# Transposes and logits moved into the last attention round; the attention's tiles laid anew over the experts' weights

## The chip, the cores and the metric

One core of one Trainium2 chip. The metric is the device time of one execution in microseconds, the median of the runs shown. The kernel before took 555.84 us (555.8 to 557.96 in three runs).

## The reference

Three layers follow one another: a linear attention with a decaying state (4 batches, 8 heads, 768 tokens, head size 48), a mixture of experts in which every slot is a weighted mean of all tokens (3072 tokens, 384 wide, 8 experts of 4 slots, 1024 hidden), and a squared-ReLU layer (2048 hidden).

```python
for t in range(S):                                   # attention, y: [B, H, S, D]
    cur = einsum('bhd,bhe->bhde', u[None] * kt, vt)
    y[:, :, t] = einsum('bhd,bhde->bhe', rt, state + cur)
    state = wt[:, :, :, None] * state + einsum('bhd,bhe->bhde', kt, vt)
x = y.transpose(0, 2, 1, 3).reshape(B * S, H * D)    # [3072, 384]
logits = x @ phi                                     # [3072, 32]
d = softmax of logits over the tokens                # max over axis 0
slot_input = (d.T @ x).reshape(E, S_per_e, D)
slot_out[e] = relu(slot_input[e] @ w1[e]) @ w2[e]
x = (softmax of logits over the slots) @ slot_out
h = relu(x @ w_in); out = (h * h) @ w_out
```

## The kernel before

The attention runs in eight rounds (`ROUNDS`), each of four heads of one batch in two sets `s` of two heads. A round turns its inputs (r, k, w) on TensorE into two banks `tbank` (`turn_inputs`, L402), which ScalarE copies out (`inputs_out`, L743); it then works in six levels per set (`level`, L451 for the levels 1 to 3, L468 for 0, 4 and 5), between which VectorE scales the tiles (`update`, L1041) and merges products (`merge`, L1063) and ScalarE widens operands (`widen`, L802). The order on every engine is written out by hand. While round `rd` works through its levels, the inputs of round `rd + 1` are turned and the rest of round `rd - 1` is finished: k turned (`turn_k`, L415; out by `k_out`, L773), k times v (`k_times_v`, L432; out by `kv_out`, L781), the scan over chunks (`scan`, VectorE, L1070), the near and the far product (`y_near`, L485; `y_far`, L501), and the copy to the tile `X` (`y_to_x`, L818). The nine `next_inputs` places of the last round are empty, since no round follows.

Behind the last level the rest of the last round stands alone. Between its steps TensorE turns x (`turn_x`, L559: 24 uses of three 128x128 transposes each, in 4 banks, evacuated by ScalarE, L891, and VectorE, L1102, in turns). Twenty uses concern columns of earlier rounds, and four need the last round. Then come the logits (L583: 24 products of 384 columns, each executed as two matmul instructions, four 32-column groups of the array side by side), their copy (L904), the maximum over tokens (L1105, turned by L594), both softmaxes, the slots (L605), the experts' first product with `w1_sb` (L623, all eight experts), and their second product in two halves: `down(0)` with `w2_lo`, `down(1)` with `w2_hi` (both L646; `down(1)` waits for a quarter of `w2_hi` before each quarter of its steps). The squared-ReLU layer (L707 to L709) takes the rest of the span.

Weights come by DMA, 1.5 MB for one expert's w1. ScalarE's queue issues `w1` (`load_w1`, L237): experts 0 to 2 in the rounds 0 to 2; experts 3 to 5 in the last round behind the first levels, and 6 and 7 at its end. SP's queue issues `w2_lo[3]` when the last y is in `X` (L335), `w2_lo[0:3]` after the logits (L337), `w_in` (L339), and `w2_hi` in 16 pieces (L343). `w1_sb` lies over the attention's tiles, so an expert can be loaded only when the tiles under it are done with. Before, behind the three early experts lie nat, rt, rk2, rk0 and wl, in this order (the end of wl0 is past expert 7); `x_t`, where the turned x goes, begins behind the eighth expert and so lies over the rest of wl0, wl1, aa0, wide, k_tok and the first of rk1, of which the last round uses several.

## Time and profile before

| | |
|---|---|
| median of three runs | 555.84 us |
| the profiled execution | 555.19 us, span 553.4 us, mean granted clock 0.953 |
| TensorE busy | 485.5 us (88%) |
| VectorE / ScalarE busy | 334.6 us (60%) / 332.8 us (60%) |
| shares of the chain that ended last | PE 72%, ACT 11%, issue 7%, SPq 4%, DVE 4% |
| attention | to about 264 us; mixture of experts to about 320 us; squared-ReLU layer to the end |

In the profile a busy share tells how long an engine had work, not what the end waited for; for that there is the chain of waits, which is followed back from the last instruction. "issue" in it is time in which an engine waited for nothing that the profile shows. The granted clock is a share of TensorE's full speed: 1.00 is 2.4 GHz and 0.50 is 1.2 GHz.

### The profile page before, as it was taken

How to read it: one execution, taken by the hardware profiler on the slowest of the kernel's cores; microseconds unless marked ns; L12 is line 12 of the kernel's file. 1: busy time of each engine (PE TensorE's matmuls, PEld its weight loads, DVE VectorE, ACT ScalarE, POOL GpSimd, SP SyncE). 2: the span in 40 equal slices, each digit the busy share in tenths (PEclk: the TensorE clock that was granted, in tenths of full speed). 3: DMA queues.
4: the chain of work that ended last, by engine and by line, in shares of the span. 5: the costliest groups of instructions: out<-in, count | busy, mean ns of one | idle time of the engine just before them, and what ended most of it. 6: DMA issues, size and time to landing. Idle time of an engine off the chain costs nothing.

```text
span 553.4 us, 18757 instructions
## 1 busy us (share of the span) xinstructions
PE 485.5 (88%) x7850; PEld 425.1 (77%) x7850; DVE 334.6 (60%) x583; ACT 332.8 (60%) x689; POOL 13.7 (2%) x21
## 2 busy tenths in 40 slices
PE   1778889798989898678698879999999999999996
PEld 0557768677777777667333469999999999999996
DVE  5688868587878788925341167555555555555552
ACT  1787677686868687434221276656565656565653
POOL 9000000000000000000000000000000000000000
PEclk9998989798989899959889979999999999999999
DMA  6885565736262621293799730101010101010101
GB/s 112 146 213 103 150 113 152 137 70 117 57 118 52 114 56 34 59 403 136 238 390 369 260 114 1 44 1 44 1 43 2 43 0 43 0 43 1 44 1 43
DMA packets 119788, 56.23 MB, mean 102 GB/s; under 512 B 102944, under 2 KB 116256, under 8 KB 119328
## 3 DMA queue, kind: packets, MB, share of 16 engines
q1 hardware_dynamic: 116512, 42.54, 31.1%
q10 hardware_dynamic: 3200, 12.58, 6.1%
q8 instruction: 60, 0.98, 0.8%
q14 instruction: 16, 0.13, 0.1%
HBM read 50.38 MB, written 4.72 MB: 100 GB/s over the span
## 4 chain that ended last, share of the span: by engine, by line
PE 72%; ACT 11%; issue 7%; SPq 4%; DVE 4%; DMA 0%; ACTq 0%; DVEq 0%
PE bank L707 12%; PE bank L708 12%; PE bank L709 12%; ACT wide L802 4%; PE ybank L485 4%; PE lbank L468 4%; PE ybank L501 4%; PE lbank L451 4%; PE bank L697 4%; SPq L289 4%; PE tbank L402 3%; PE tbank L415 2%; PE bank L646 2%; PE bank L623 2%; ACT wl L743 2%
## 5 line engine op out<-in xcount | busy, mean ns | idle before, releaser
L707 PE MATMUL bank<-wo_high,h_high 128*128 128x384 f32 x384 | 129.6, 337 | 1.8 <-DVE h_low L1207 1.6
L708 PE MATMUL bank<-wo_low,h_high 128*128 128x384 f32 x384 | 129.0, 336 | 0.0
L709 PE MATMUL bank<-wo_high,h_low 128*128 128x384 f32 x384 | 128.9, 336 | 0.0
L953 ACT ACTIVATE h_relu<-bank 128x384 f32<-128x384 f32 x128 | 62.9, 492 | 74.4 <-PE bank L697 74.1
L1205 DVE CAST h_high<-h_sq 128x384 fp32r<-128x384 f32 x128 | 46.0, 359 | 96.7 <-PE bank L709 88.0
L1041 DVE TENSOR_TENSOR rk<-rk,wl 112x768 f32<-112x768 f32 x80 | 76.3, 954 | 36.7 <-PE lbank L468 19.9
L707 PEld LDWEIGHTS bank<-wo_high,h_high 128*128 128x128 f32 x384 | 72.6, 189 | 3.2 <-issue 2.7
L1207 DVE TENSOR_TENSOR h_low<-h_sq,h_high 128x384 fp32r<-128x384 f32 x128 | 71.5, 558 | 4.5
L708 PEld LDWEIGHTS bank<-wo_low,h_high 128*128 128x128 f32 x384 | 72.7, 189 | 0.0
L709 PEld LDWEIGHTS bank<-wo_high,h_low 128*128 128x128 f32 x384 | 72.5, 189 | 0.0
L957 ACT ACTIVATE h_sq<-h_relu 128x384 f32<-128x384 f32 x128 | 67.4, 527 | 4.1
L1063 DVE COPY_PREDICATED aa<-masks,lbank 128x384 f32<-128x384 int32 (+1 forms) x80 | 59.8, 748 | 10.4 <-PE lbank L468 10.3
L402 PE MATMUL tbank<-ident,nat 128*112 128x128 f32 x288 | 50.0, 296 | 12.3 <-ACT wl L743 6.9
L451 PE MATMUL lbank<-wide,rk 128*64 128x64 f32 x1152 | 45.0, 228 | 10.6 <-ACT wide L802 9.6
L802 ACT ACTIVATE wide<-rk 48x384 f32<-48x384 f32 x96 | 51.1, 533 | 5.2 <-DVE rk L1041 3.3
L451 PEld LDWEIGHTS lbank<-wide,rk 128*64 128x64 f32 x1152 | 39.0, 140 | 19.2 <-issue 14.0
L402 PEld LDWEIGHTS tbank<-ident,nat 128*112 128x112 f32 x288 | 30.4, 138 | 23.5 <-ACT wl L743 7.9
L697 PE MATMUL bank<-c_st,m_st 128*128 (+1 forms) x126 | 42.7, 339 | 0.3 <-ACT h_relu L953 0.3
L501 PE MATMUL ybank<-kv,rk 64*64 64x48 f32 x768 | 22.8, 266 | 10.0 <-issue 9.9
L818 ACT ACTIVATE xs<-ybank 128x288 f32<-128x288 f32 x32 | 11.4, 408 | 31.4 <-PE ybank L501 31.4
L485 PE MATMUL ybank<-v_tok,aa 64*64 64x48 f32 x768 | 25.9, 219 | 1.7 <-issue 1.7
L468 PEld LDWEIGHTS lbank<-rk 64*32 64x32 f32 (+1 forms) x1536 | 21.8, 126 | 7.0 <-issue 4.9
(123 smaller groups left out, 532.5 us busy)
## 6 DMA issues: line engine op xcount, KB each, us to landing
w_sb<-in_moe_w_dram ACTq DMA_DIRECT2D x8, 1536.0 KB, 8.7
w_hi<-in_moe_w_dram SPq DMA_DIRECT2D x16, 384.0 KB, 8.0
nat<-in_w_dram SPq DMA_DIRECT2D x64, 72.0 KB, 2.4
nat<-in_r_dram SPq DMA_DIRECT2D x64, 72.0 KB, 2.5
nat<-in_k_dram SPq DMA_DIRECT2D x64, 72.0 KB, 2.4
v_tok<-in_v_dram SPq DMA_DIRECT2D x32, 144.0 KB, 3.1
w_lo<-in_moe_w_dram SPq DMA_DIRECT2D x1, 4608.0 KB, 16.8
out_dram<-o_sb SPq DMA_DIRECT2D x8, 576.0 KB, 3.0
```

Source lines behind the costliest of these rows:

```text
L402: last = nc.tensor.transpose(bank[0:TOK, g * P:(g + 1) * P], nat[s][:, x, at:at + TOK], ident[:])
L451: last = nc.tensor.matmul(dst[:, :, SUB * i:SUB * i + SUB], src[:, 1, C * c:C * c + C], wide[s][:, :, SUB * c:SUB * c + SUB], start=True, ...
L697: nc.tensor.matmul(h_bank[fb % 2][:, 0:GT * P], m_st[:, fb * P:(fb + 1) * P], c_st[:, bass.ds(g * (GT * P), GT * P)], start=True, stop=Tru ...
L707: nc.tensor.matmul(acc, hi, wo_high[:, fb, :], start=(fb == 0), stop=False)
L708: nc.tensor.matmul(acc, hi, wo_low[:, fb, :], start=False, stop=False)
L709: last = nc.tensor.matmul(acc, lo, wo_high[:, fb, :], start=False, stop=(fb == NF - 1))
L802: nc.scalar.activation(wide[s][a:b, h, :].rearrange("p (n m) -> p n m", m=m), right, ACT.Copy)\
L953: nc.scalar.activation(h_relu[fb % 2][:], h_bank[fb % 2][:, 0:GT * P], ACT.Relu).then_inc(relu_done, 1)
L957: nc.scalar.activation(h_sq[fb % 2][:], h_relu[fb % 2][:], ACT.Square).then_inc(sq_done, 1)
L1041: nc.vector.tensor_tensor(scaled_half(rk[rd % 3][s], m), scaled_half(rk[rd % 3][s] if lv else rt[s], m), by, ALU.mult).then_inc(updated[s], 1)
L1063: nc.vector.copy_predicated(dst, mask, data).then_inc(merged[s], 1)
L1207: nc.vector.tensor_tensor(h_low[i][:], h_sq[i][:], h_high[i][:].bitcast(F32), ALU.subtract)\
```

## The change

Eighteen of the 24 uses of x are turned in the nine `next_inputs` places of the last round, in the two banks `tbank`, and evacuated by ScalarE alone (1, 2, 3, 3, 1, 2, 3, 1 and 2 of them, in this order; the inputs had 1, 1, 2, 2, 1, 1, 2, 1 and 1). Two more follow `turn_k`, and four come behind the last y, as before. The logits of the first three batches are computed in two halves, one before and one after `y_near` of set 0; those of the last batch behind the last y, in three 32-column groups of 256 columns. The maximum is taken in two parts and combined. To make room, the attention's tiles are laid anew: wl, rk0, aa0, wide, k_tok and v_tok now lie under the experts 3 to 7, and nat, rt, rk2 under `x_t`. Expert 3 is loaded at the start of the last round, the experts 4 to 6 behind its last update (in front of `k_out`), and expert 7 behind the last `y_to_x`. `lt` moves behind `m_parts`, and `w2_lo[0:3]` is issued after the third part of the logits.

The parts of the diff below are, in this order, the constants and the tiles, TensorE's program (`next_inputs`, `logits`, the tail), ScalarE's, and SP's.

```diff
-    X_EARLY = (2 * D * 2 * (ROUNDS - 1)) // P
+    X_EARLY = 2 * ((2 * PW * (ROUNDS - 2)) // P)
+    X_NEXT = 2 * ((2 * PW * (ROUNDS - 1)) // P)
...
         sb("w1_early", [P, W1_EARLY, KB, FF], c=att)
+        wl = [sb(f"wl{b}", [P, 2, W_LEN], c=att) for b in range(2)]
+        rk0 = [sb(f"rk0_{s}", [P, 2, S], c=att) for s in range(2)]
+        aa0 = [sb(f"aa0_{s}", [P, NB, C], c=att) for s in range(2)]
+        wide = [sb(f"wide{s}", [P, 2, S // 2], c=att) for s in range(2)]
+        k_tok = [sb(f"k_tok{s}", [P, PER, 112], c=att) for s in range(2)]
+        v_tok = [[sb(f"v_tok{s}{b}", [P, PER, 2, D], c=att) for b in range(1 + s)] for s in range(2)]
         nat = [sb(f"nat{s}", [P, 3, PER * TOK], c=att) for s in range(2)]
...
+            def turn_block(n, dst):
+                rs, half = divmod(n, 2)
+                for i in range(GT):
+                    src = X[:, GT * half + i].rearrange("p r n -> p (r n)")[:, rs * P:(rs + 1) * P]
+                    last = nc.tensor.transpose(dst[:, i * P:(i + 1) * P], src, ident[:])
+                return last
...
             def next_inputs(rd, first, count):
                 if rd < ROUNDS - 1:
                     turn_inputs(rd + 1, first, count)
+                else:
+                    for s in range(2):
+                        pe.wait_ge(y_evac[s], 2 * (ROUNDS - 2))
+                    for n in range(3 * first // 2, 3 * (first + count) // 2):
+                        turn_block(n, bank_for(t_use["x", n])).then_inc(t_full, 1)
...
+            def logits(half):
+                for kb in range(KB):
+                    for b in range(B - 1):
+                        last = nc.tensor.matmul(bank[4 + half][SL * b:SL * b + SL, 0:384], phi_sb[:, kb, :],
+                                                xt_view(2 * (KB * b + kb) + half), start=(kb == 0), stop=(kb == KB - 1))
+                last.then_inc(logit_mm, 1)
-            turn_x(0, 4)
+            turn_x(X_EARLY, X_NEXT)
             k_times_v(ROUNDS - 1, 0)
             k_times_v(ROUNDS - 1, 1)
-            turn_x(4, 12)
+            pe.wait_ge(phi_loaded, 16)
+            logits(0)
             y_near(ROUNDS - 1, 0)
+            logits(1)
             y_far(ROUNDS - 1, 0)
-            turn_x(12, 2 * X_EARLY)
             y_near(ROUNDS - 1, 1)
             y_far(ROUNDS - 1, 1)
             after_attention(pe)
-            turn_x(2 * X_EARLY, XT_USES)
...
+            turn_x(X_NEXT, XT_USES)
+            for kb in range(KB):
+                for q in range(3):
+                    last = nc.tensor.matmul(bank[6][SL * q:SL * q + SL, 0:2 * P], phi_sb[:, kb, :],
...
+                                            start=(kb == 0), stop=(kb == KB - 1))
+            last.then_inc(logit_mm, 1)
...
             for rd in range(ROUNDS):
+                if rd == ROUNDS - 1:
+                    for s in range(2):
+                        act.wait_ge(updated[s], 6 * rd)
+                    act.wait_ge(w_pair, 6 * rd)
+                    for s in range(2):
+                        act.wait_ge(w_spread[s], rd)
+                    load_w1(act, W1_EARLY, W1_EARLY + 1)
...
-                if rd == ROUNDS - 1:
-                    for s in range(2):
-                        act.wait_ge(updated[s], 6 * rd + 2)
-                    load_w1(act, W1_EARLY, NE - 2)
...
-                if rd == ROUNDS - 1:
-                    load_w1(act, NE - 2, NE)
+            for s in range(2):
+                act.wait_ge(updated[s], 6 * ROUNDS)
+                act.wait_ge(y_mm[s], ROUNDS - 1)
+            load_w1(act, W1_EARLY + 1, NE - 1)
             for s in range(2):
                 k_out(ROUNDS - 1, s)
-            x_out(0, 4)
+            x_out(X_EARLY, X_NEXT)
             kv_out(ROUNDS - 1, 0)
             kv_out(ROUNDS - 1, 1)
-            x_out(4, 12)
             for half in range(2):
                 act.wait_ge(logit_mm, half + 1)
+                nc.scalar.activation(lt[0:LAST, half * 384:(half + 1) * 384], bank[4 + half][0:LAST, 0:384], ACT.Copy)\
                     .then_inc(lt_copy, 1)
             y_to_x(ROUNDS - 1, 0)
-            x_out(12, 2 * X_EARLY)
             y_to_x(ROUNDS - 1, 1)
+            load_w1(act, NE - 1, NE)
             after_attention(act)
-            x_out(2 * X_EARLY, XT_USES)
+            x_out(X_NEXT, XT_USES)
+            act.wait_ge(logit_mm, 3)
+            nc.scalar.activation(lt_last[0:LAST], bank[6][0:LAST, 0:2 * P], ACT.Copy).then_inc(lt_copy, 1)
...
-            sp.wait_ge(logit_mm, 2)
+            sp.wait_ge(logit_mm, 3)
             sp.dma_start(w2_lo[:, 0:3], w2_v[:, 0:3]).then_inc(w2_lo_loaded, 16)
```

In the places of the last round ScalarE copies the turned x out of `tbank` (`next_out`, with a wait for level 0 and its update of both sets ahead of the first).

## Rows read from the trace of the kernel before

**Rows 1.** Chain of waits, 232 to 314 us (start us, length us, what).
```profile
232.58 1.71 issue
...
237.79 3.10 issue
...
241.57 0.84 PE lbank L468 x48
...
242.85 0.51 ACTq L237
...
243.45 0.46 ACT k_tok L773
...
245.40 2.56 PE bank L559 x12
...
249.13 0.73 ACT kv L781 x2
...
250.00 0.76 PE ybank L432 x43
...
251.56 1.36 DVE kv L1070
...
254.62 1.55 PE ybank L485 x48
...
257.47 2.77 PE bank L559 x24
...
261.84 1.25 PE ybank L501 x48
...
263.97 0.86 PE bank L559 x6
...
266.21 4.11 PE bank L583 x48
...
271.88 0.28 PE bank L594
...
308.15 5.34 PE bank L646 x64
```

**Rows 2.** Windows (us, busy us of PE, PEld, DVE, ACT, POOL; clock, DMA share, GB/s).
```profile
163.30:185.40 22.10, 20.83 (x657) 17.73 (x659) 18.55 (x26) 16.13 (x37) 0.00 (x0) 0.98 0.43 79
...
218.60:242.40 23.80, 16.22 (x619) 14.73 (x618) 15.17 (x19) 9.90 (x22) 0.00 (x0) 0.86 0.44 157
...
237.00:249.00 12.00, 8.54 (x164) 7.49 (x156) 2.86 (x4) 5.15 (x12) 0.00 (x0) 0.50 1.04 401
...
264.00:272.00 8.00, 6.54 (x67) 3.70 (x67) 2.07 (x3) 1.85 (x4) 0.00 (x0) 1.00 0.68 203
...
272.00:310.00 38.00, 32.42 (x288) 14.30 (x291) 13.77 (x35) 9.33 (x16) 0.00 (x0) 0.91 1.04 372
```

**Rows 3.** Timeline, ScalarE's queue at 231 us, and one evacuation of x.
```profile
231.90 1.33 ACTq L237 DMA_DIRECT2D w_sb<-in_moe_w_dram  x1
...
233.26 1.12 ACTq L237 DMA_DIRECT2D w_sb<-in_moe_w_dram  x1
...
252.57 0.49 ACT L891 ACTIVATE x_t<-bank 128x384 f32<-128x384 f32 x1 [0.16 <-PE bank L559]
```

**Rows 4.** Timeline, TensorE after the loads of experts 1 and 2.
```profile
70.36 0.24 PE L501 MATMUL ybank<-kv,rk 64*64 64x48 f32 x1 [2.52 <-issue]
...
99.90 0.56 PE L501 MATMUL ybank<-kv,rk 64*64 64x48 f32 x10 [3.21 <-issue]
```

**Rows 5.** Part 3 of the page, the instruction queue (packets, MB, share of 16 engines).
```profile
q8 instruction: 60, 0.98, 0.8%
```

**Rows 6.** Timeline, TensorE in round five (start, length, engine, line, operation).
```profile
163.31 1.21 PE L451 MATMUL lbank<-wide,rk 128*64 128x64 f32 x24
...
170.71 0.86 PE L402 MATMUL tbank<-ident,nat 128*112 128x128 f32 x6
...
174.29 0.54 PE L402 MATMUL tbank<-ident,nat 128*112 128x128 f32 x3
```

More of the change, by code:

```diff
@@ L58, in fused_kernel @@
                 count_use((rd_n + 1, s, x, half), T_EVACS[x][half])
+        if rd_n == ROUNDS - 1:
+            for n in range(X_EARLY):
+                count_use(("x", n), 1)
     ctx = ExitStack()
@@ L555, in turn_x @@
                     wait_xt_bank(pe, n)
-                    rs, half = divmod(n, 2)
-                    for i in range(GT):
-                        src = X[:, GT * half + i].rearrange("p r n -> p (r n)")[:, rs * P:(rs + 1) * P]
-                        last = nc.tensor.transpose(bank[n % 4][:, i * P:(i + 1) * P], src, ident[:])
-                    last.then_inc(xt_full, 1)
+                    turn_block(n, bank[(n - X_EARLY) % 4]).then_inc(xt_full, 1)
+            def logits(half):
[4 more added lines that the diff above has]
+                last.then_inc(logit_mm, 1)
             for s in range(2):
@@ L766, in inputs_out, with next_out @@
                     input_out(rd, s, x, half)
+            def next_out(rd, first, count):
+                if rd < ROUNDS - 1:
+                    inputs_out(rd + 1, first, count)
+                else:
+                    if first == 0:
+                        for s in range(2):
+                            act.wait_ge(level_mm[s], 6 * rd + 1)
+                            act.wait_ge(updated[s], 6 * rd + 1)
+                    for n in range(3 * first // 2, 3 * (first + count) // 2):
+                        evac(t_use["x", n], xt_view(n), tbank[t_use["x", n] % 2][:, 0:384])
             def k_out(rd, s):
@@ L875, in _ @@
                     y_to_x(rd - 1, 1)
-                if ahead:
-                    inputs_out(rd + 1, 11, 1)
+                next_out(rd, 11, 1)
                 if ahead:
```

110 lines of the change are left out of this document (50 added, 60 removed).

## The prediction

> **What bounds the kernel now.** The shares of the chain that ended last come first, in the table above: TensorE holds 72% of it and "issue" 7%. TensorE is the bound, but not evenly, so the chain in order of time is read next, for the place that the change touches. Between 232 and 242 us it shows two stretches in which TensorE waits for nothing visible, 1.71 and 3.10 us, the second inside the far product of set 1 [rows 1]. The windows tell what is going on there: from 237 to 249 us the DMA engines are at 1.04 of their share with 401 GB/s, and the granted clock is 0.50, that is 1.2 GHz [rows 2]; ScalarE's queue had just issued three experts [rows 3]. Two single-expert loads in earlier rounds are followed by stalls of 2.52 and 3.21 us of the same kind [rows 4]. Instructions come by DMA too, 60 packets and 0.98 MB in all, 16 KB each [rows 5]. I read these stalls as TensorE's program arriving late behind weights. From the last level (end at 242.41) to the last y in `X` (263.97) go 21.6 us; then 7.9 to the turned maximum (271.88) [rows 1]. Last, I ask what follows: from 272 to 310 us the DMA engines are at 1.04 without a break, 372 GB/s for 38.0 us [rows 2]. That is 14.1 MB, all of w2_lo[0:3], w_in and w2_hi (4.7 + 3.1 + 6.3). The last quarter of w2_hi is wanted at 308.15 + 3/4 of 5.34 = 312.2 us [rows 1], so it arrives only 2 us ahead of its use.
>
> **The last round, up to its last level.** Expert 3's issue on ScalarE, ahead of `k_out`, costs between 0 and 0.5 us (one issue, 0.51 [rows 1]): I take 0.3. The stretch from level 1 of set 0 to the last level now takes 23.7 us (218.71 to 242.41), of which TensorE is busy 16.2 and VectorE 15.2; the same stretch of round five, with the inputs of another round in the gaps, takes 22.1, of which TensorE is busy 20.8 [rows 2]. Its first product ran at the low clock (1.21 for the 0.92 of the others at full clock) [rows 6], so 21.8 is its length at full clock. The changed last round is like it, but with 18 uses in place of 12, and in blocks of 2 and 3 in place of 1 and 2. One use alone is 0.54 long, two together 0.86 [rows 6]: a second costs some 0.36. A third waits until ScalarE has emptied the first of only two banks (0.49 each [rows 3]), and I take 0.6. Three blocks grow from one to two, three from two to three, the others stay: 3 x 0.36 + 3 x 0.6 = 2.9 us. VectorE has no next round to prepare, which should give back half of TensorE's 1.3 us of idle time: -0.5. So 21.8 + 2.9 - 0.5 = 24.2, which is 0.5 more than now although the two stalls (4.8 us) are gone. The bounds are -0.7 (all idle time recovered, 0.4 for each of six uses) and +1.5. Expert 3's own load lasts some 4 us (1.57 MB at 401 GB/s) and can stall TensorE as those of experts 1 and 2 did, 0 to 3.2 us; round 0's load left none that long, and no input loads run beside this one, so I take 0.4. Sum for the round: +1.2 us.
>
> **From the last level to the last y.** Count from the level's end, now 242.41. VectorE's last update ends about 1.0 later. Only then may ScalarE issue experts 4 to 6, three in a row, and `k_out` stands behind them on its queue; TensorE's second `turn_k` waits for `k_out`, and k times v for that. At 231 us the second and third issue took 1.33 and 1.12 [rows 3]; the pair at 242 went at 0.51 each [rows 1]. Three are 1.5 to 3.0 us; I take 2.2, so `k_out` begins at 3.2 and not, as now, at 1.0. Then `k_out` of set 0 until 4.0, turned k 0.4, two uses of x (6 of the 24 transposes that take 2.77 [rows 1]) 0.7, k times v 0.8: 5.9. kv_out 0.73: 6.7. k times v of set 1 0.8 with its wait: 7.5. Half the logits: three batches side by side take the steps of four, 4.11 / 2 = 2.05 each [rows 1]: 9.6, under which kv_out (0.75) and most of the scan (1.36) go. y_near 1.6: 11.2; second half of the logits 2.05: 13.2; y_far 1.25: 14.5. The copy to `X` takes 0.87 with its waits (263.09 to 263.97), and the near product of set 1 waits for it, since the eight uses of x (2.77) that covered it are gone: 15.4. Near, far and copy once more: 19.1. Now it is 21.6, so -2.5 (bounds -3.2 and -1.7 by the issues). Of the logits so moved only about 1 us is hidden. Against this stand the late instructions: experts 4 to 6 are 4.7 MB or 12 us of full DMA engines, from about 245 us on, over some 230 matmuls. Before, five experts (7.9 MB, some 20 us at 401 GB/s) gave stalls of 4.8 us. I take 1.2 us (0 to 4.8), and 0.5 (0 to 2) for the lower clock that `k_out`'s wait and the stalls may bring; the current tail also runs its first 7 us at 0.50 [rows 2], which my steps, at full clock, have already taken away. Sum: -0.8 us.
>
> A page of the Trainium skill speaks against such stalls: "Runtime: NRT & Kernel Launch", section "Instruction fetch mechanics", says that programs come in 16 KiB blocks of 256 instructions and that the cost of crossing a block is mostly hidden. The size agrees with [rows 5]; the stalls of [rows 1, 4] do not look hidden. What the trace would give if it held is the last rival.
>
> **Behind the last y.** The four uses of x stay (2.24 from 263.97 to 266.21). The logits shrink from 4.11 to six steps of 256 columns, 6 x 4.11 / 12 x 2/3 = 1.4. From their end to the turned maximum it is 1.56 now (270.32 to 271.88) with a copy and a maximum over 768 columns; over 256 and with a combination I take 1.1. That is 4.7 in place of 7.9: -3.2 us for all that TensorE does up to `down(1)`.
>
> But the DMA engines do not get shorter work there, they get more: expert 7 (1.57 MB) now starts with `w2_lo[3]` at the last y. Now the 8.0 us from 264 to 272 move 203 GB/s, or 1.6 MB [rows 2], and then come the full 38.0. After it both go together, 3.15 MB at 401 GB/s, 7.8 us, some 1.5 us after the issue, and w2_lo[0:3] joins without a gap: 1.5 + 7.8 + 38.0 = 47.3 us after the last y, for the last quarter of w2_hi. Its use would come at 48.2 - 3.2 = 45.0. `down(1)` so waits some 2.3 us, and ends at 47.3 + 1.3 = 48.6 in place of 49.5 (313.49 - 263.97): -0.9 us remain of the 3.2 (bounds -3.2 and -0.2). A slower clock in between costs nothing as long as this wait exists.
>
> **Sum.** +1.2 - 0.8 - 0.9 = -0.5 us on the profiled execution's 555.19, 554.7; the median of the runs shown lies 0.65 above that, so 555.3 us.
>
> **Rivals.**
> *The weights come in time.* The queue's latency or the rate behind the last y is better than my sum, or the slots' part slows enough; the 3.2 us remain whole. For it: the wait that I foresee is only 2.3 us. Against: [rows 2] show no gap to gain in. -0.5 - 2.3 = -2.8: 553.0 us.
> *Instructions late behind experts 4 to 6 (slower).* The place is from `k_out` to the near product of set 0. There the steps are a chain of short waits between TensorE and ScalarE, and about two blocks of program are crossed while 12 us of weights are queued. The price is that of the two stalls at 232 and 237 us, 4.8 instead of 1.2, and 1.8 instead of 0.5 for the clock at 0.50: +4.9, so +4.4 and 560.2 us. It decides once the stalls in the tail sum to over 4 us. For it: every load of [rows 1, 4] had such a stall. Against: from 243 to 251 us, with the DMA engines as full, no step was longer than the clock explains by more than 1 us.
> *Instructions are not held up by weights.* What the two stalls before were is then something else that goes with the old order; the 0.4, 1.2 and 0.5 fall away: -2.6, 553.2 us. "DMA: Bandwidth & Descriptors" of the Trainium skill, "Queues, rings and completion order", has each engine take turns between its queues packet by packet, which would let a program block through early; the stalls of [rows 4], behind single loads, speak against it.
>
> **How the numbers follow.** A difference of 0.5% or 2.8 us is about what can be told from none. The forecast has 0.38, and of itself lies between 552.8 and 558.0; the weights in time 0.30; late instructions 0.17; no hold-up 0.15. Faster by over 0.5%: 0.055 + 0.18 + 0 + 0.085 = 0.32. Slower: 0.055 + 0 + 0.135 + 0 = 0.19. Within: 0.49. The range 550.6 to 559.2 takes in both faster cases with their bounds and part of the slow one; beyond lies a case with all bounds on one side.
>
> **What would show it.** In the changed trace, the last round should have no idle TensorE over 2 us between 219 us and its last level, which should end near 243.6; L237 should stand between the last update and `k_out` for some 2 us; the last y should be in `X` near 264.4, the DMA share should be 1.0 from some 2 us after it for 45 us, and TensorE should wait inside the second half of L646 for a DMA. If `down(1)` runs through in 5.34 us, the second step of my sum behind the y is wrong. If the stretch from level 1 to the last level is under 23 us, the uses of x were cheaper than 0.36 to 0.6. If the last y comes before 262 us or after 267, the tail is wrong.

## The result, and the profile after

The changed kernel took 561.25 us (median of eleven runs, 559.28 to 565.35), the kernel before 555.8 in as many. The ratio is 1.0107, with a 95% interval of 1.0085 to 1.0129: about 1% slower, where 0.1% faster was forecast.

The profiled execution has a span of 559.1 us, 5.7 more than before. The page's first line and its chain of waits by engine:

```profile
span 559.1 us, 18790 instructions
...
PE 69%; ACT 13%; issue 6%; DVE 3%; SPq 3%; POOL 2%; DMA 2%; ACTq 1%; DVEq 0%; POOLq 0%
```

TensorE's share of the chain fell from 72% to 69%, and a DMA stands in the chain with 2%, where before it was 0%. The chain in order of time says where (start, length, what):

```profile
216.30 0.37 ACTq L246
...
220.68 2.72 issue
...
224.48 1.48 PE lbank L460 x24
...
225.96 1.15 PE ybank L441 x44
...
249.66 0.37 ACTq L246
...
250.07 0.51 ACTq L246
...
250.61 0.51 ACTq L246
...
251.16 0.46 ACT k_tok L808
...
256.92 2.07 PE bank L582 x18
...
260.51 2.07 PE bank L582 x18
...
262.58 1.23 PE ybank L510 x48
...
263.83 0.72 ACT xs L853 x2
...
268.54 0.86 PE bank L519 x6
...
273.39 0.26 PE bank L618
...
306.88 9.70 DMA w_hi<-in_moe_w_dram
...
316.62 2.83 PE bank L670 x16
```

These answer to [rows 1]. Expert 3 is issued at 216.30, and 4.4 us later TensorE stands still for 2.72 us, in the middle of k times v. The steps behind the stall are slow: the level takes 1.48 us for the usual 0.85. The three issues of experts 4 to 6 (249.66 to 251.12) stand right in front of `k_out`, and the two halves of the logits (256.92 and 260.51) are in the chain at their full 2.07. The last y is in `X` at 268.40. Then comes the line that was forecast: the chain waits for w2_hi until 316.6. But the last quarter of `down(1)` behind it takes 2.83 us and not the 1.3 of my sum.

Windows of the changed kernel (columns as in [rows 2]): the stretch from level 1 of set 0 to the last level, the time behind the stall, the tail up to the last y, and the transfers behind it.

```profile
219.35:248.50 29.15, 24.33 (x672) 20.66 (x672) 15.71 (x19) 17.38 (x40) 0.00 (x0) 0.94 0.16 51
...
222.00:228.00 6.00, 4.60 (x98) 3.90 (x97) 2.19 (x4) 3.07 (x8) 0.00 (x0) 0.72 0.03 10
...
248.50:268.40 19.90, 14.85 (x334) 10.69 (x334) 5.18 (x5) 7.05 (x18) 0.00 (x0) 0.91 0.62 240
...
272.00:316.50 44.50, 36.13 (x326) 15.74 (x320) 14.32 (x37) 9.70 (x17) 0.00 (x0) 0.92 1.06 383
```

The first was 23.8 us with TensorE busy 16.2 [rows 2]; it is 29.1 with 24.3. The tail went from 21.5 to 19.9. Behind it the DMA engines are full for the whole 44.5 us to w2_hi's last byte, where they were for 38.0 before.

The timeline of TensorE shows what a third use of x in one gap costs, and where `down(1)` stops:

```profile
231.67 0.88 PE L519 MATMUL tbank<-ident,xs 128*128 128x128 f32 x6
...
233.09 0.55 PE L519 MATMUL tbank<-ident,xs 128*128 128x128 f32 x3 [0.54 <-ACT x_t L767]
...
309.84 4.08 PE L670 MATMUL bank<-w_hi,h_t 128*32 128x384 f32 x48
...
316.62 2.79 PE L670 MATMUL bank<-w_hi,h_t 128*32 128x384 f32 x16 [2.69 <-DMA w_hi<-in_moe_w_dram]
```

The third use (233.09) waits 0.54 us for ScalarE to empty a bank. Three quarters of `down(1)` run in 4.08 us; the last waits 2.69 us for the DMA and then runs 2.79.

The span falls into five stretches, here for the profile of every kernel: up to level 1 of set 0 in the last round (A), from there to the last level (B), to the last y in `X` (C), to the first product of the last layer (D), and to the end (E), in us.

| kernel | A | B | C | D | E | ratio to before (95%) |
|---|---|---|---|---|---|---|
| before | 218.6 | 23.7 | 21.5 | 60.2 | 229.3 | |
| changed | 219.4 | 29.1 | 19.9 | 61.6 | 229.1 | 1.0107 (1.0085 to 1.0129) |
| e1, expert 3 later | 221.1 | 24.9 | 19.9 | 60.5 | 229.1 | 1.0032 (0.9994 to 1.0071) |
| e2, w_in behind w2_hi | 216.8 | 29.1 | 20.0 | 62.4 | 228.9 | 1.0144 (1.0059 to 1.0229) |
| e3, without expert 7 | 220.1 | 29.1 | 22.4 | 57.7 | 229.5 | 1.0074 (1.0034 to 1.0114) |
| e4, loads alone | 218.1 | 23.6 | 23.6 | 60.3 | 229.2 | 1.0050 (1.0015 to 1.0085) |
| e5, expert 3 in pieces | 219.7 | 26.1 | 22.5 | 61.8 | 229.1 | 1.0052 (1.0007 to 1.0098) |
| e6, k_out first | 221.2 | 28.7 | 19.9 | 61.7 | 229.3 | 1.0085 (1.0043 to 1.0127) |
| e7, expert 7 early | 223.2 | 29.6 | 19.6 | 57.2 | 229.3 | 1.0076 (1.0035 to 1.0116) |
| e8, logits in waits | 218.6 | 29.1 | 20.0 | 61.7 | 228.9 | 1.0108 (1.0012 to 1.0204) |
| e9, SP issues | 219.8 | 30.3 | 18.5 | 60.2 | 229.2 | 1.0074 (1.0043 to 1.0106) |
| e10, two per gap | 220.7 | 26.7 | 22.4 | 61.6 | 229.3 | 1.0135 (1.0092 to 1.0178) |
| e11, together | 218.4 | 25.5 | 17.6 | 58.8 | 229.6 | 0.9991 (0.9961 to 1.0022) |
| e12, before, in pieces | 222.6 | 23.0 | 21.4 | 59.4 | 230.2 | 0.9989 (0.9958 to 1.0020) |
| e13, four edits | 220.2 | 25.0 | 19.5 | 60.4 | 229.3 | 0.9975 (0.9935 to 1.0016) |
| e14, five edits | 221.7 | 23.8 | 18.5 | 57.2 | 228.8 | 0.9942 (0.9902 to 0.9983) |

A varies from 216.8 to 223.2 among kernels whose program is the same there, so one span says little here. Each row is one execution, and that one can lie far from the median (in e2 558.89 us, with a median of 564.23). Seven kernels share the program of B: it is 29.1 in the changed kernel, e2, e3 and e8, and 28.7, 29.6 and 30.3 in e6, e7 and e9. C is 19.9 in the changed kernel and 22.4 in e3, with the same program. So a difference of 1 us in B to D tells something only when the clock is looked at beside it.

### The profile page after: what moved, and what is told of

It reads as the page before. It is cut to its first block, busy times and chain, and to the rows that moved or that the text cites. A ratio compares the mean times of both kernels' runs of the same rounds, so it can differ in the third digit from the quotient of the medians.

```text
span 559.1 us, 18790 instructions
## 1 busy us (share of the span) xinstructions
PE 491.1 (88%) x7858; PEld 425.4 (76%) x7858; DVE 331.0 (59%) x576; ACT 336.6 (60%) x699; POOL 13.6 (2%) x21
## 3 DMA queue, kind: packets, MB, share of 16 engines
q1 hardware_dynamic: 116512, 42.54, 30.3%
## 4 chain that ended last, share of the span: by engine, by line
PE 69%; ACT 13%; issue 6%; DVE 3%; SPq 3%; POOL 2%; DMA 2%; ACTq 1%; DVEq 0%; POOLq 0%
PE bank L731 12%; PE bank L733 12%; PE bank L732 12%; PE lbank L460 6%; ACT wide L837 5%; PE ybank L494 4%; PE tbank L411 4%; PE bank L721 4%; PE ybank L510 4%; SPq L352 3%; PE lbank L477 2%; PE ybank L441 2%; DMA w_hi<-in_moe_w_dram 2%; POOL rk L388 1%; ACT wl L767 1%
## 5 line engine op out<-in xcount | busy, mean ns | idle before, releaser
L1073 DVE TENSOR_TENSOR rk<-rk,wl 112x768 f32<-112x768 f32 x80 | 76.2, 952 | 43.7 <-PE lbank L460 24.2
L411 PE MATMUL tbank<-ident,nat 128*112 128x128 f32 x288 | 52.2, 307 | 11.2 <-ACT wl L767 6.7
L460 PE MATMUL lbank<-wide,rk 128*64 128x64 f32 x1152 | 46.3, 231 | 7.3 <-ACT wide L837 6.4
L411 PEld LDWEIGHTS tbank<-ident,nat 128*112 128x112 f32 x288 | 31.8, 143 | 22.9 <-ACT wl L767 7.6
L477 PEld LDWEIGHTS lbank<-rk 64*32 64x32 f32 (+1 forms) x1536 | 21.4, 122 | 8.2 <-issue 6.3
L477 PE MATMUL lbank<-rk 64*32 64x32 f32 (+1 forms) x1536 | 25.2, 210 | 2.2 <-DVE aa L1095 1.7
```

The lines of the kernel that those rows point to most:

```text
L411: last = nc.tensor.transpose(bank[0:TOK, g * P:(g + 1) * P], nat[s][:, x, at:at + TOK], ident[:])
L460: last = nc.tensor.matmul(dst[:, :, SUB * i:SUB * i + SUB], src[:, 1, C * c:C * c + C], wide[s][:, :, SUB * c:SUB * c + SUB], start=True, ...
L1073: nc.vector.tensor_tensor(scaled_half(rk[rd % 3][s], m), scaled_half(rk[rd % 3][s] if lv else rt[s], m), by, ALU.mult).then_inc(updated[s], 1)
```

## The experiments

The theory after the result: the change loses in three places, all about DMA. Expert 3's load holds TensorE's program up in the last round; the issues of experts 4 to 6 stand in ScalarE's queue on the path; and the bytes behind the last y set the end of `down(1)`. The rival: the eighteen uses of x in the last round cost what the round grew by.

**e1: expert 3 later.**

```diff
-                if rd == ROUNDS - 1:
-                    for s in range(2):
-                        act.wait_ge(updated[s], 6 * rd)
-                    act.wait_ge(w_pair, 6 * rd)
-                    for s in range(2):
-                        act.wait_ge(w_spread[s], rd)
-                    load_w1(act, W1_EARLY, W1_EARLY + 1)
...
             for s in range(2):
                 k_out(ROUNDS - 1, s)
+            load_w1(act, W1_EARLY, W1_EARLY + 1)
```

> The changed kernel, with expert 3 loaded behind k_out of the last round, after experts 4 to 6, instead of at the round's start. Theory (program blocks late behind a load): the stall of 2.72 us inside k times v at 220.7 us and the stretch at 0.58 of the clock behind it go, the stretch from level 1 of set 0 to the last level shrinks from 29.1 to some 25.2 us, and as 1.6 MB more now lie in the idle of the DMA engines before the last y, nothing is lost there: about 557.4 us, 3.5 to 4 under the changed kernel. Rival (the eighteen uses of x cost what the round grew by): the stretch stays above 28 us and the time near 561.

Measured: 558.31 us, ratio 1.0032. B is 24.9 us, and its window shows the full clock throughout:

```profile
221.07:246.00 24.93, 22.69 (x672) 19.36 (x672) 15.71 (x19) 17.27 (x40) 0.00 (x0) 1.00 0.07 15
```

So one load of 1.57 MB, put on top of the moved work, costs 4.2 us: the stall of 2.7 and the slow steps behind it. Nothing was lost in the tail (19.9), where a stall of 1.07 us showed. The rival, a stretch of over 28 us without the load, is refuted. That does not make 4.2 of the 5.4 us the load's alone: e4 below has the load without the moved work, and its stretch is 23.6. It is long only with both.

What the stall waits for can be read too. The trace lists every packet of the instruction queue, 16 KB each ([rows 5] has their sum). In the changed kernel the 41st of 60 is moved from 220.95 to 221.88 us, and TensorE goes on at 223.40, 1.5 us after its end. Of the stalls of 0.6 us or more that the sixteen profiles put down to "issue" between 20 and 312 us, 131 of 135 end in this way, 1.2 to 1.7 us after the end of such a packet; three of the other four stand right behind the last y. So these stalls are TensorE's program arriving. And the load delays it:

| expert 3 in the last round | start of the 41st packet, from the start of level 1 |
|---|---|
| not loaded there (before, e1, e12) | 1.4 us ahead of it |
| in three pieces (e5, e11, e13, e14) | 0.2 to 0.5 us ahead of it |
| in one piece (the changed kernel, e2 to e4, e6 to e10) | 1.4 to 1.9 us behind it |

The transfer of expert 3 runs from 2.0 us ahead of level 1 to about 4 us behind it. The packet itself takes 0.9 to 1.0 us in all sixteen; what moves is its start, by some 3 us. Why it starts later is not in the trace.

**e2: w_in behind w2_hi.** The two lines that issue w_in move behind the loop over w2_hi.

```diff
-            sp.wait_ge(slot_mm, 1)
-            sp.dma_start(w_in_sb[:], w_in.rearrange("(k p) n -> p k n", p=P)).then_inc(w_in_loaded, 16)
             sp.wait_ge(up_mm, 2)
...
+            sp.wait_ge(slot_mm, 1)
+            sp.dma_start(w_in_sb[:], w_in.rearrange("(k p) n -> p k n", p=P)).then_inc(w_in_loaded, 16)
             sp.wait_ge(ct_full, CT_USES)
```

> The changed kernel, with SP issuing w_in behind the 16 pieces of w2_hi instead of ahead of them. Theory (behind the last y the sum of bytes sets the end, and in the order w_in, w2_hi the wait falls inside down(1), with four products still behind it): down(1) runs through in about 5.4 us, w_in's last bytes land where w2_hi's did, near 48 us after the last y, and the product with w_in (L703) waits for them instead. It began 52.5 us after the last y and should begin near 49: about 4 us gained, 557.3 us. Rival (the wait in down(1) was itself caused by something else, for instance its issue): no gain, and the wait stays at the same place.

Measured: 564.23 us (four runs), ratio 1.0144; D is 62.4 and not 58. `down(1)` ran through in 5.5 us, as expected. But the product with w_in began only 51.6 us after the last y (317.39 - 265.82), and slowly:

```profile
317.39 4.55 PE L703 MATMUL bank<-w_in_sb,slot_ot 128*32 128x512 f32 x24 [4.94 <-issue]
```

It takes 4.55 us where before it took 2.83. w_in's transfer was complete at 317.30, so it is what the product waited for, though the view says "issue". The place of the wait moved as foreseen, the gain didn't come. w2_hi may be issued only when half of the experts' first product is done (287.96), and until then the queue now ran dry: the DMA share was 0.66 from 286 to 290 us, with 203 GB/s. That was w_in's place, and my expectation had left it out.

**e3: without expert 7.**

```diff
-            load_w1(act, NE - 1, NE)
...
-            pe.wait_ge(w1_loaded, 16 * NE)
+            pe.wait_ge(w1_loaded, 16 * (NE - 1))
...
-                                                    w1_sb[:, 4 * grp + j, kb, 512 * half:512 * half + 512],
+                                                    w1_sb[:, min(4 * grp + j, NE - 2), kb, 512 * half:512 * half + 512],
```

> The changed kernel without the load of expert 7; the first expert product takes expert 6's weights in its place, so the load of 1.57 MB is left out and all else is as it was. Theory (bytes behind the last y): the transfers end 3.9 us earlier, w2_hi is complete some 44 us after the last y, down(1) does not wait (2.69 us) and does not run its last quarter at the low clock (1.4 us): 557.1 us. Rival (the wait comes from the late start of w2_lo[0:3] or of w2_hi, not from the bytes): less than 1 us is gained.

Measured: 560.77 us, ratio 1.0074. D is 57.7 us, the 3.9 less of the expectation. `down(1)` still waits 1.44 us, but its last quarter runs at the full clock, in 1.50 us. The profiled execution did not gain in all, because its C was 22.4: from 252 to 262 us the granted clock was 0.50. So the bytes behind the last y are what `down(1)` waits for. The last quarter starts 45.5 us after the last y instead of 48.2; of the 4.0 us by which `down(1)` ends sooner 2.7 are the earlier bytes, and 1.3 the full clock behind a shorter wait. The loss of 2.5 us in the tail has nothing to do with the edit, since e5 and e10 show it too.

**e4: the loads alone.** The kernel before with the new order of tiles and the new times of `load_w1` (as in the change's diff), the transposes and logits as they were.

```diff
+                if rd == ROUNDS - 1:
...
+                    load_w1(act, W1_EARLY, W1_EARLY + 1)
...
-                if rd == ROUNDS - 1:
-                    for s in range(2):
-                        act.wait_ge(updated[s], 6 * rd + 2)
-                    load_w1(act, W1_EARLY, NE - 2)
...
-                if rd == ROUNDS - 1:
-                    load_w1(act, NE - 2, NE)
+            for s in range(2):
+                act.wait_ge(updated[s], 6 * ROUNDS)
+                act.wait_ge(y_mm[s], ROUNDS - 1)
+                act.wait_ge(w_spread[s], ROUNDS)
+            load_w1(act, W1_EARLY + 1, NE - 1)
+            for s in range(2):
                 k_out(ROUNDS - 1, s)
...
             y_to_x(ROUNDS - 1, 1)
+            load_w1(act, NE - 1, NE)
```

> The kernel before with the changed kernel's layout of tiles and its times of the loads of experts 3 to 7, but with the turning of x and the logits where they were before. It splits the change in two. Theory: the last round has the stall behind expert 3 (2.7 us and its slow clock) in place of the two of 4.8 us, about 23 us from level 1 to the last level; k_out begins 1.6 us later behind three issues; the tail runs at full clock; behind the last y the 7.9 us up to the turned maximum stay, so w2_hi (complete 48 us after the last y) is just in time for down(1). Sum -1 to -2 on the kernel before: 554.3 us, so that the whole loss of the change lies in what was moved, 7 us. Rival (the loads are what costs): above 558.

Measured: 559.49 us, ratio 1.0050: 2.8 us slower than the 556.64 of the kernel before, run beside it, not 1 to 2 faster. B and D came as expected (23.6 and 60.3), C did not: 23.6 us. TensorE, with what its waits ended with:

```profile
221.92 0.47 PE L432 MATMUL ybank<-v_tok,k_tok 64*48 64x48 f32 x21 [2.53 <-issue]
...
236.38 2.18 PE L485 MATMUL ybank<-v_tok,aa 64*64 64x48 f32 x47 [1.25 <-issue]
...
245.04 1.35 PE L415 MATMUL tbank<-ident,rk 112*128 112x112 f32 x6 [2.05 <-ACT k_tok L773]
```

The stall behind expert 3 is there (2.53), and another of 1.25; from that one on, about 237 us, the clock is at 0.50 until about 254 us, through the wait for `k_out` (2.05, with the three issues in it). So about half of the loss (2.8 of 5.4 us; by the interval 0.8 to 4.7) comes from the new load times alone. The moved work adds the rest: it makes B 5.5 us longer (23.6 to 29.1), C 3.7 shorter, some of which is the clock, and D 1.3 longer. In B, the load costs nothing against the kernel before, whose two stalls (4.8 us) are gone in turn, and 4.2 us with the moved work in the gaps. In the kernel before TensorE waits 0.35, 0.95 and 1.37 us for ScalarE between the first levels; in e4 0.47 and 0.39 are left of this, so a part of the stall falls where TensorE would have waited anyway. In the changed kernel the gaps are full. How much was hidden is not shown, since two stalls went at the same time.

**e5: expert 3 in three pieces.**

```diff
+            def load_piece(i):
+                act.dma_start(w1_sb[:, W1_EARLY, i], w1_v[W1_EARLY][:, i]).then_inc(w1_loaded, 16)
...
-                    load_w1(act, W1_EARLY, W1_EARLY + 1)
+                    load_piece(0)
...
                 next_out(rd, 2, 2)
+                if rd == ROUNDS - 1:
+                    load_piece(1)
...
                 next_out(rd, 6, 1)
+                if rd == ROUNDS - 1:
+                    load_piece(2)
```

> The changed kernel, with expert 3 loaded in three pieces of 0.5 MB at three places of the last round (its start, behind the third and the sixth group of x) instead of in one of 1.57 MB. Theory (TensorE's next block of program waits behind what is queued, and the stall comes when that takes longer than the block before it runs): 1.3 us of transfers at a time hold no block up, so no stall of over 1 us and no stretch at 1.2 GHz, and the stretch from level 1 of set 0 to the last level is 25 us as without the load (24.9), not 29.1: the time near 557.5. Rival (any load in the round costs its bytes, in one piece or three): 27 us or more.

Measured: 559.01 us, ratio 1.0052. B is 26.1, nearer to the 24.9 without the load than to 29.1. One stall is left, at the same place:

```profile
221.82 0.48 PE L441 MATMUL ybank<-v_tok,k_tok 64*48 64x48 f32 x21 [0.76 <-issue]
```

0.76 us where it was 2.72, and the clock stays at 1.00. The rival (a cost by bytes, 27 us or more) is refuted here. The time was 559.0 and not 557.5; C was 22.5, again with the clock at 0.50, from 250 to 258 us.

**e6: k_out first.**

```diff
-            load_w1(act, W1_EARLY + 1, NE - 1)
             for s in range(2):
                 k_out(ROUNDS - 1, s)
+            load_w1(act, W1_EARLY + 1, NE - 1)
```

> The changed kernel, with k_out of both sets ahead of the issue of experts 4 to 6 on ScalarE. Theory: the three issues (1.45 us) leave the path, k_out begins about 1.1 us after the last level and not 2.7; the tail of 19.9 us up to the last y becomes 18.3 or less, and TensorE's wait of 2.0 us before its second turn_k is under 1. As w2_hi still lands some 48 us after the last y, the gain stays: 559.5 us. Rival (the issue runs beside the update and costs nothing): the tail stays at 19.9.

Measured: 560.53 us, ratio 1.0085; C is unchanged, 19.9. The wait did not go, it moved:

```profile
251.67 0.77 PE L424 MATMUL tbank<-ident,rk 112*128 112x112 f32 x6 [0.76 <-ACT k_tok L808]
...
256.01 0.76 PE L441 MATMUL ybank<-v_tok,k_tok 64*48 64x48 f32 x44 [2.25 <-ACT kv L816]
```

TensorE waits 0.76 us for `k_out` in place of 2.0, and then 2.25 in place of 0.92 for kv_out, which now stands behind the three issues. My theory had named `k_out` and forgotten the next one in the queue.

**e7: expert 7 early.**

```diff
-        v_tok = [[sb(f"v_tok{s}{b}", [P, PER, 2, D], c=att) for b in range(1 + s)] for s in range(2)]
+        rk2_1 = sb("rk2_1", [P, 2, S], c=att)
...
-        rk2 = [sb(f"rk2_{s}", [P, 2, S], c=att) for s in range(2)]
+        rk2 = [sb("rk2_0", [P, 2, S], c=att), rk2_1]
+        v_tok = [[sb(f"v_tok{s}{b}", [P, PER, 2, D], c=att) for b in range(1 + s)] for s in range(2)]
...
             kv_out(ROUNDS - 1, 1)
+            load_w1(act, NE - 1, NE)
...
-            load_w1(act, NE - 1, NE)
```

> The changed kernel, with v_tok and rk2 of set 1 changing places, so that nothing but k_tok is still in use under expert 7, and expert 7 issued behind kv_out of set 1 instead of behind the last y. Theory (the bytes behind the last y set the end): its 1.57 MB go before the last y, and w2_hi is complete some 44.5 us after it, so down(1) waits under 0.5 us or, as with expert 7 left out, 1.4 us at most: from the last y to the first product of the last layer 57.7 us in place of 61.6, and 557.3 us if the tail stays at 19.9; the load may stall a block in the tail by 1 to 2.5 us, which would take half of it back. Rival: no gain behind the y.

Measured: 560.53 us, ratio 1.0076. D is 57.2 (57.7 expected), C 19.6. The last quarter of `down(1)`:

```profile
317.39 1.50 PE L671 MATMUL bank<-w_hi,h_t 128*32 128x384 f32 x16 [2.35 <-DMA w_hi<-in_moe_w_dram]
```

`down(1)` ends 46.6 us after the last y instead of 51.0, as in e3 (47.0), here with nothing left out. The time was expected at 557.3 and is 560.53. The median shows less of the gain than the profile's D does; A was 223.2 in this profile, and that spread hides what an edit gains.

**e8: the logits in the waits.**

```diff
...
+            pe.wait_ge(phi_loaded, 16)
             k_times_v(ROUNDS - 1, 0)
+            pe.wait_ge(t_evac, t_out[t_use["k", ROUNDS - 1, 1, 1]])
+            logits(0, (0,))
             k_times_v(ROUNDS - 1, 1)
-            logits(0)
+            logits(0, (1, 2))
             y_near(ROUNDS - 1, 0)
-            logits(1)
             y_far(ROUNDS - 1, 0)
+            logits(1, (0, 1, 2))
...
-            y_to_x(ROUNDS - 1, 0)
+                if half == 0:
+                    y_to_x(ROUNDS - 1, 0)
             y_to_x(ROUNDS - 1, 1)
```

> The changed kernel, with the logits put where TensorE waits anyway: the first third of the first half between the two k times v (a wait of 0.92 us for kv_out), and the second half behind the far product of set 0, where y_near of set 1 waits 0.93 for the copy. Theory: the tail up to the last y is 19.9 - 0.7 - 0.9 = 18.3 us, the time 559.6. Rival (the tail hangs on something else, the scan or ScalarE): 19.9 or more.

Measured: 561.15 us (four runs), ratio 1.0108; C is 20.0, no gain. The waits went (0.16 for kv_out), but two stalls of 0.56 and 0.64 us came inside the near products, 1.3 and 1.4 us after the end of an instruction packet: what the steps gained, they lost for the most part to a program that did not come sooner. The clock was at 0.58 for four of the twenty, as in the changed kernel's tail. With one profile, it stays open whether the edit would gain without the stalls.

**e9: SP issues experts 4 to 6.**

```diff
+            for s in range(2):
+                sp.wait_ge(updated[s], 6 * ROUNDS)
+                sp.wait_ge(y_mm[s], ROUNDS - 1)
+                sp.wait_ge(w_spread[s], ROUNDS)
+            load_w1(sp, W1_EARLY + 1, NE - 1)
...
             for s in range(2):
-                act.wait_ge(updated[s], 6 * ROUNDS)
-                act.wait_ge(y_mm[s], ROUNDS - 1)
-            load_w1(act, W1_EARLY + 1, NE - 1)
-            for s in range(2):
                 k_out(ROUNDS - 1, s)
```

> The changed kernel, with experts 4 to 6 issued by SP's queue, which waits for the same events, instead of by ScalarE. The transfers begin at the same time. Theory (the three issues stand in ScalarE's queue, before k_out or, as the run with k_out first showed, before kv_out): k_out begins 1.1 us after the last level instead of 2.7, kv_out follows k times v at once, and the tail up to the last y is some 1.5 us shorter than 19.9 (or than 22.4, where it runs at 1.2 GHz). Rival (the issue is hidden by the update and by TensorE's own work): under 0.3 us.

Measured: 559.7 us, ratio 1.0074. C is 18.5, 1.4 less; the wait of 2.0 us before the second `turn_k` is 0.38 here, and that for kv_out is 0.91. Some of the 1.4 is the clock, at 1.00 in this tail, and against it stand two stalls of 0.79 and 0.39 us. e1 is the cleaner partner, with the same three issues in ScalarE's queue and full clock: its wait is 1.99, so 1.6 us go. With e6 this shows that the issues themselves were on the path. (B was 30.3: the stall was 2.95 and the clock at 0.50 for six us behind it.)

**e10: two uses per gap.**

```diff
+    EVEN = {f: (2 * i, 2 * i + 1) for i, f in enumerate((0, 1, 2, 4, 6, 7, 8, 10, 11))}
...
-                    for n in range(3 * first // 2, 3 * (first + count) // 2):
+                    for n in EVEN[first]:
```

> The changed kernel, with two uses of x in each of the nine gaps of the last round instead of 1, 2, 3, 3, 1, 2, 3, 1 and 2. Theory (a third use in a gap waits for ScalarE, 0.54 to 0.94 us four times in the trace, since there are two banks only): the waits go, 0.6 us each for three gaps, and the stretch from level 1 of set 0 to the last level goes from 29.1 to 27.5 us, the stall behind expert 3 still in it. Rival (TensorE then waits for the levels instead): 29.

Measured: 562.0 us (four runs), ratio 1.0135. B is 26.7, with a stall of 2.53 in it, and TensorE's waits for `x_t` are gone from it. The clock was at 0.57 for four us behind the stall, as in the changed kernel, so it is not the reason for the 2.4 us. The time did not follow (C was 22.4, at 0.50). e14 below against e11 repeats the gain in B (23.8 for 25.5).

**e11: together.** The edits of e5, e7 and e9, with SP also issuing expert 7 (behind `kv_mm` of both sets), and experts 0 to 2 in nine pieces:

```diff
+            def early_piece(i):
+                if i < W1_EARLY * KB:
+                    act.dma_start(w1_sb[:, i // KB, i % KB], w1_v[i // KB][:, i % KB]).then_inc(w1_loaded, 16)
...
                 next_out(rd, 4, 2)
+                early_piece(2 * rd)
                 widen(rd, 1, 3)
+                early_piece(2 * rd + 1)
...
-                if rd < W1_EARLY:
-                    load_w1(act, rd, rd + 1)
```

> The changed kernel with everything that the runs point to: expert 3 in three pieces in the last round; v_tok and rk2 of set 1 in changed places, so that expert 7 can go before the last y; experts 4 to 7 issued by SP's queue; and experts 0 to 2 in nine pieces of 0.5 MB in the middle of the rounds 0 to 4, where the input loads rest, instead of whole in the rounds 0 to 2. Theory: against the changed kernel -3 in the last round, -1.5 in the tail, -4 behind the last y, and -5 for the stalls of 2.5 us each in the rounds 1 and 2 and the slow clock behind them: -10 to -13, some 549 us, 1.2% under the kernel before. Rival (pieces delay the program as much as whole experts do): the stalls stay and the time is near 556.

Measured: 554.7 us, ratio 0.9991 to the kernel before (556.0 beside it). B to D are 101.9 us, against 110.6 of the changed kernel and 105.4 of the kernel before. The three terms of the last round, the tail and behind the y came at 3.6, 2.3 and 2.8; the 5 us of the early rounds did not come. The stalls there:

```profile
72.31 0.24 PE L519 MATMUL ybank<-kv,rk 64*64 64x48 f32 x1 [1.27 <-issue]
...
99.77 0.50 PE L519 MATMUL ybank<-kv,rk 64*64 64x48 f32 x10 [0.85 <-issue]
```

**e12: the kernel before with experts 0 to 2 in pieces.** The last edit alone.

```diff
                 widen(rd, 0, 3)
                 if ahead:
                     inputs_out(rd + 1, 4, 2)
+                early_piece(2 * rd)
                 widen(rd, 1, 3)
+                early_piece(2 * rd + 1)
...
-                if rd < W1_EARLY:
-                    load_w1(act, rd, rd + 1)
```

> The kernel before, with experts 0 to 2 loaded in nine pieces of 0.5 MB in the middle of the rounds 0 to 4 and nothing else changed. Theory (a block of program waits behind what is queued; a piece passes before the block is wanted): the stalls of 2.52 us at 70 us and 3.21 us at 100 us go, with some 1 us of low clock: 551 us. Rival (the stalls belong to the input loads, or the program is late there anyway): within 1 us of 556.

Measured: 555.76 us, ratio 0.9989: no gain, the rival's case.

```profile
62.86 0.54 PE L402 MATMUL tbank<-ident,nat 128*112 128x128 f32 x3 [0.86 <-issue]
...
67.28 1.02 PE L485 MATMUL ybank<-v_tok,aa 64*64 64x48 f32 x28 [0.73 <-issue]
...
72.03 0.24 PE L501 MATMUL ybank<-kv,rk 64*64 64x48 f32 x1 [1.54 <-issue]
...
92.88 0.41 PE L501 MATMUL ybank<-kv,rk 64*64 64x48 f32 x9 [1.39 <-issue]
...
101.22 0.51 PE L501 MATMUL ybank<-kv,rk 64*64 64x48 f32 x10 [0.84 <-issue]
```

In place of two stalls of 2.5 and 3.2 us [rows 4] there are five, of 0.7 to 1.5, 5.4 us in all. The pieces are moved from 57.8 to 62.4 us and from 87.5 to 92.3, so only the instruction packets of the first and the fourth stall (60.46 and 90.52) start beside a piece. Those of the other three start 2 to 7 us after the last piece, when nothing but inputs is moved. There the rival's second half holds: the program is late anyway. That a part of the stalls of [rows 4] was not the weights' doing either follows only if these are the same stalls, which is not shown.

**e13 and e14: four and five edits.** e13 is e11 with the gaps of e10 and with experts 0 to 2 whole; e14 has their pieces too. e14 against e11, and e13 against e14:

```diff
+    EVEN = {f: (2 * i, 2 * i + 1) for i, f in enumerate((0, 1, 2, 4, 6, 7, 8, 10, 11))}
...
-                    for n in range(3 * first // 2, 3 * (first + count) // 2):
+                    for n in EVEN[first]:
```

```diff
-                early_piece(2 * rd)
                 widen(rd, 1, 3)
-                early_piece(2 * rd + 1)
...
+                if rd < W1_EARLY:
+                    load_w1(act, rd, rd + 1)
```

> The changed kernel with expert 3 in three pieces, the changed places that let expert 7 go early, experts 4 to 7 issued by SP's queue, and two uses of x in each gap; experts 0 to 2 whole, as in the kernel before. Theory: the last round 24.5 us (25.5 in the combination before, less 1 for the third uses), the tail 17.6, behind the last y 58.8, and the first rounds as they were, since pieces there gained nothing: some 1 us better than the combination run before, 554 us, 2 to 2.5 under the kernel before. Rival (the pieces of experts 0 to 2 did give some 2 us): 556.

> The same with experts 0 to 2 in nine pieces in the rounds 0 to 4 as well. Theory (in the early rounds beside the input loads, pieces delay the program as much in sum as the whole experts, as the kernel before with pieces showed): as the kernel without them, within 1 us, 554 us. Rival (they give 2 us): 552.

Measured: 555.08 us (0.9975) and 552.12 us (0.9942, 0.9902 to 0.9983), against 555.99 of the kernel before run beside them. e13 lies between its theory (554) and its rival (556), and its profile misses in every stretch (25.0, 19.5 and 60.4 for 24.5, 17.6 and 58.8), with the clock at 0.50 from 262 to 280 us. e14 has the number of its rival (552) and not of its theory. B to D are 104.9 and 99.5. In e14 the last round has 23.8 us with all eighteen uses of x in it, and `down(1)` ends 46.5 us after the last y. e14 is the only version whose whole interval lies below the kernel before: 0.6% faster, and 1.6% under the ratio of the change. It is the best of fourteen, and the interval ends at 0.9983, so that it is faster at all rests on little. The two intervals overlap, so whether the pieces of experts 0 to 2 help is left open: the stalls at 71 and 99 us are 1.54 and 0.77 with them and 2.83 and 3.19 without, but A is not smaller (221.7 and 220.2).

## Why the prediction was wrong

Against the profiled execution, step by step (us):

| step | forecast | profile |
|---|---|---|
| issue of expert 3, up to level 1 | +0.3 | +0.7, with the spread of A in it |
| uses of x in the last round, stalls of before gone | +0.5 | +1.2 (e1: 24.9 for 23.7) |
| expert 3's load in the last round | +0.4 | +4.2 (29.1 against e1's 24.9) |
| tail up to the last y | -0.8 | -1.6 |
| behind the last y | -0.9 | +1.4 |
| the last layer | 0 | -0.2 |
| sum | -0.5 | +5.7, as the spans |

**The step that failed** is the cost of expert 3's load in the last round: "0 to 3.2 us; round 0's load left none that long, and no input loads run beside this one, so I take 0.4". It is 3.8 of the 6.2 us between forecast and profile. The kind of stall was right and its size wrong. Two of three loads of the same size had stalls of 2.5 and 3.2 us [rows 4], and I took a value near the one that had none. The stall came at 2.5 to 3.1 in every one of nine profiles with the whole load in the last round. And its cost, 4.2 us, lies outside even the bounds, because I had priced it without the clock: the 1.2 GHz behind it cost another 1.3 us (1.48 for 0.85 and 1.15 for 0.76 in the chain, and the x beside them). That no input loads run beside it holds (the last of v is moved just ahead of it), but did not help.

I had also misread a line that this rests on. The first of the two stalls before (232.58 to 234.28 [rows 1]) is not behind weights: its instruction packet was moved from 231.50 to 232.77 us, ahead of the first packet of the weights at 232.89. The program is late without weights elsewhere too: near 160 and 190 us, where none are moved, every one of the sixteen profiles has a stall of 0.75 to 2.0 us.

**Behind the last y**, the other 2.3 us, the mechanism was right: bytes, not products, set the end. w2_hi arrived 48.2 us after the last y (47.3 forecast), and `down(1)` waited 2.7 us (2.3). e3 and e7 confirm it from the other side: with 1.57 MB less behind the last y its last quarter starts 2.7 and 3.2 us sooner, and `down(1)` ends 4.0 and 4.4 us sooner. What failed is the sentence that a slower clock costs nothing as long as the wait exists. It costs nothing ahead of the wait: in e1 the slots' part took 2.8 us less than in the changed kernel and `down(1)` only ended 1.1 sooner. But the wait of 2.7 us is itself followed by 1.2 GHz, so the last quarter took 2.79 and not 1.3. That is chance in part: in e9 a wait of 2.71 us was followed by a quarter of 1.50.

**The tail** came better than its term. The last y came at 268.4, which my own sign (after 267) would count against the tail; but it is the round that was late. The issues cost 1.45 us and not 2.2, and in the changed kernel no stall of over 0.4 us came in it, though three experts were in flight from 250.7 to 264.5 us. (e1, e7, e8 and e9 have stalls of 0.4 to 1.1 us there.) My terms for it (1.2, and 4.8 in the rival) came from another misreading: the 4.8 us of [rows 1] are said to stem from five experts, but experts 6 and 7 were issued at 242.85, after both stalls. The near product of set 1 does wait for the copy (0.93), and the logits are in the chain at their full length, as forecast. The rival of late instructions in the tail did not occur, though its time, 560.2, is near the measured one; the same mechanism struck one place earlier, behind a single expert.

**The uses of x.** Without the load the stretch is 24.9 us (e1), 0.7 more than my 24.2. This is partly luck. A third use does wait for its bank, as assumed, for 0.54 to 0.94 us, but its own 0.5 comes on top: it costs 1.1 to 1.3 us in the changed kernel and not the 0.6 of my term. Three of them are 1.7 us more than forecast; what gave 1.0 of it back is not shown. (By [rows 6] a second use costs 0.86 - 0.54 = 0.32 us and not 0.36, which changes little.)

**The rivals.** "Instructions are not held up by weights" is refuted: with the whole load in the round the packet of the next instructions starts some 3 us later than without, and TensorE's stall ends 1.5 us after the packet does. By that rule of the Trainium skill ("Runtime: NRT & Kernel Launch", "Instruction fetch mechanics"), the cost of crossing a block is mostly hidden; the trace agrees for most of the 60 packets of the changed kernel, and does not for the seven that end in a stall of 0.6 us or more, the one beside expert 3 among them. "The weights come in time" did not occur.

## What to carry to other kernels

Weights that cost nothing by their bytes can still hold up the program. Here 1.5 MB in one piece, issued inside a stretch that TensorE bounds, cost 4.2 us, the same in 0.5 MB pieces 1.2 us, and an issue 0.5 us of the engine that issues it. Look for the instruction packets in the trace when TensorE stands still for nothing visible. Before filling a gap with work, ask what it hides and what runs out behind it: once the products are short, the bytes still to come set the end, and a shorter step ahead of them gains nothing. A stall on TensorE should be priced with the slow steps that may follow it, here 1.3 us behind one of 2.7.

## What was not expected of the hardware

The same wait can be followed by either clock. TensorE's wait for `k_out` in e1 and in e10:

```profile
249.25 0.77 PE L424 MATMUL tbank<-ident,rk 112*128 112x112 f32 x6 [1.99 <-ACT k_tok L808]
```

```profile
250.67 1.35 PE L425 MATMUL tbank<-ident,rk 112*128 112x112 f32 x6 [1.99 <-ACT k_tok L809]
```

After 1.99 us of waiting in both, the six transposes take 0.77 us in the one and 1.35 in the other, and the tail that follows is 19.9 us in the one and 22.4 in the other. The programs of the two differ ahead of this wait (in the gaps) and by one more load behind it in e1. The changed kernel and e3 have the same program up to the last y, and there the tail is 19.9 us in the one, with the clock at 0.50 to about 255 us, and 22.4 in the other, with 0.50 to 262. This is 2.5 us of difference without a difference in the program. It may be a good part of the spread between executions; with one trace of each kernel that is not shown.

The row of the granted clock can miss slow steps. TensorE at the start, in the changed kernel and in e2, whose program is the same there:

```profile
17.31 2.38 PE L411 MATMUL tbank<-ident,nat 128*112 128x128 f32 x9 [0.45 <-ACT rk L767]
```

```profile
17.32 0.95 PE L411 MATMUL tbank<-ident,nat 128*112 128x128 f32 x6 [0.43 <-ACT rk L767]
```

Nine input transposes take 2.38 us in the one, 0.26 each, with the clock shown at 1.00, and six take 0.95 in the other, 0.16 each.
